# Two matrix products on TensorE in 64-row halves instead of 128 rows

## What is computed

```python
w = softmax(weight_gen, axis=-1)                  # per token and head, 7 taps
x_pad = zeros of 6 tokens, then x
out = einsum('bshk,bskhg->bshg', w, the 7 tokens up to s)
x = out.reshape(B * S, D)
h = x @ w_in                                      # 16384 x 192 by 192 x 2048
g = h * clip(h + 3.0, 0.0, 6.0) / 6.0
return g @ w_out                                  # 16384 x 2048 by 2048 x 192
```

## Time and profile before

| | us |
|---|---|
| median of 3 runs | 1226.28 |
| lowest and highest | 1226.02, 1226.76 |
| span of the profiled execution (first to last instruction) | 1224.4 |
| TensorE matmuls busy | 1194.6 (98%) |
| TensorE weight loads busy | 1083.3 (88%) |
| VectorE busy | 803.7 (66%) |
| ScalarE busy | 634.2 (52%) |
| GpSimd busy | 690.8 (56%) |

### The profile page before, as it was taken

How to read it: one execution, slowest core, us unless ns; L and a number is a source line. 1 busy time by engine, 2 the same in 40 slices (tenths; PEclk the granted TensorE clock), 3 DMA queues, 4 the chain that set the end, 5 groups by cost and what they waited for, 6 DMA issues and landing times.

```text
span 1224.4 us, 19650 instructions
## 1 busy us (share of the span) xinstructions
PE 1194.6 (98%) x6848; PEld 1083.3 (88%) x6848; DVE 803.7 (66%) x1362; ACT 634.2 (52%) x1269; POOL 690.8 (56%) x455
## 2 busy tenths in 40 slices
PE   1999999999999999999999999999999999999998
PEld 1899999999999999999999999999999999998997
DVE  7866657576665766656666575766657666566665
ACT  3455555455555555545555554555555555455554
POOL 7893854909358192762918549094581927729100
PEclk9999999999999999999999999999999999999999
DMA  6101010010101001010010100101010010100000
GB/s 179 46 22 58 20 45 13 20 58 20 58 0 65 14 20 58 0 65 13 20 58 20 45 13 20 58 20 58 0 56 22 20 58 0 65 13 13 13 14 13
DMA packets 12071, 42.08 MB, mean 34 GB/s; under 512 B 1183, under 2 KB 5279, under 8 KB 10139
## 3 DMA queue, kind: packets, MB, share of 16 engines
q1 hardware_dynamic: 12059, 41.93, 9.8%
HBM read 29.34 MB, written 12.58 MB: 34 GB/s over the span
## 4 chain that ended last, share of the span: by engine, by line
PE 96%; DVE 1%; POOL 1%; issue 0%; DMA 0%; ACT 0%; DVEq 0%; ACTq 0%
PE work L464 48%; PE sums L482 32%; PE sums L484 15%; PE work L444 2%; POOL pool_acc L154 0%; POOL pool_prod L152 0%; DVE w_in L404 0%; DMA w_raw<-weight_gen_dram 0%; DVE work L350 0%; DVE w_out L410 0%; DVE g_lo L361 0%; DVE out_stage L381 0%; POOL pool_acc L147 0%; POOL pool_prod L148 0%; DVE xt_b L373 0%
## 5 line engine op out<-in xcount | busy, mean ns | idle before, releaser
L350 DVE SCALAR_TENSOR_TENSOR work<-relu,work 128x512 f32<-128x512 f32 x512 | 355.2, 694 | 402.9 <-ACT relu L254 402.8
L482 PE MATMUL sums<-w_out,g_hi 128*128 128x384 f32 x2048 | 614.1, 356 | 0.7 <-DVE g_lo L361 0.7
L254 ACT ACTIVATE relu<-work 128x512 f32<-128x512 f32 x512 | 306.4, 598 | 554.0 <-PE work L464 549.3
L484 PE MATMUL sums<-w_out,g_lo 128*128 128x192 f32 x2048 | 513.0, 251 | 0.0
L464 PE MATMUL work<-xt_a,w_in 128*128 128x512 f32 x1536 | 449.3, 400 | 2.0 <-DVE xt_b L373 2.0
L482 PEld LDWEIGHTS sums<-w_out,g_hi 128*128 128x128 f32 x2048 | 384.3, 188 | 23.7 <-DVE g_lo L361 1.3
L484 PEld LDWEIGHTS sums<-w_out,g_lo 128*128 128x128 f32 x2048 | 389.8, 190 | 15.8
L361 DVE TENSOR_TENSOR g_lo<-work,g_hi 128x512 fp32r<-128x512 f32 x512 | 349.7, 683 | 2.1
L464 PE MATMUL work<-xt_b,w_in 128*128 128x512 f32 x1024 | 318.1, 392 | 0.0
L264 ACT CAST g_hi<-work 128x512 fp32r<-128x512 f32 x512 | 299.3, 585 | 11.4 <-DVE work L350 11.3
L147 POOL TENSOR_TENSOR pool_acc<-x_in,w_soft 128x768 f32<-128x768 f32 (+1 forms) x32 | 50.0, 1563 | 442.7 <-DVE w_soft L341 429.7
(11 more groups left out here) (31 smaller groups left out, 203.7 us busy)
## 6 DMA issues: line engine op xcount, KB each, us to landing
x_in<-x_dram SPq DMA_DIRECT2D x15, 1344.0 KB, 6.0
out_dram<-out_stage SPq DMA_DIRECT2D x32, 384.0 KB, 2.8
w_raw<-weight_gen_dram SPq DMA_DIRECT2D x16, 224.0 KB, 3.0
w_out_raw<-moe_w_out_dram SPq DMA_DIRECT2D x1, 1152.0 KB, 13.5
x_in<-x_dram SPq DMA_DIRECT2D x1, 768.0 KB, 5.1
w_in_raw<-moe_w_in_dram SPq DMA_DIRECT2D x1, 768.0 KB, 8.9
w_in_raw<-moe_w_in_dram SPq DMA_DIRECT2D x2, 384.0 KB, 10.3
w_out_raw<-moe_w_out_dram SPq DMA_DIRECT2D x1, 384.0 KB, 6.6
```

Source lines behind the costliest of these rows:

```text
L254: nc.scalar.activation(t.relu[:, m % 2, :], t.work[m % BANKS][:], ACT.Relu, bias=3.0).then_inc(s.relu_ready, 1)
L350: nc.vector.scalar_tensor_tensor(bank[:], t.relu[:, m % 2, :], 6.0, bank[:], ALU.min, ALU.mult).then_inc(s.gated, 1)
L482: nc.tensor.matmul(t.sums[n][:, 0:2 * D], t.g_hi[:, m % BANKS, cols], t.w_out[:, j, :], start=(j == 0), stop=False)
L484: ins = nc.tensor.matmul(t.sums[n][:, D:2 * D], t.g_lo[:, m % BANKS, cols], t.w_out[:, j, 0:D], start=False, stop=(j == TILES - 1))
```

## The change

TensorE works in halves of 64 rows: each matmul takes 64 of the 128 rows of both operands, the upper (0 to 63) or the lower (64 to 127). Upper and lower matmuls alternate and write different PSUM banks. Slots go in twos, a *duo* d being slots 2d and 2d + 1. For each duo TensorE does:

- `fill_first`: five rounds of (upper half of the even tile, lower half of the odd tile);
- `multiply` of two half tiles (`parts_after` lists which: part 0 and part 1 of a tile are its two halves of rows, in each of the four token blocks);
- `fill_second`: five rounds of (upper half of the odd, lower half of the even tile);
- `multiply` of the next two half tiles.

The fifth product of a fill, the low part of `w_in` for channels 128 to 191, takes only the 256 columns in which the half of rows holds the high part of x; the product of the two low parts is left out. In `multiply`, four matmuls work on two token blocks: 384 columns upper, 384 lower, 192 upper, 192 lower. A semaphore `turned` makes a `multiply` wait until the one before has ended, `filled_first` makes the second filling of a bank wait for the first. `g_hi` and `g_lo` get 6 places instead of 4. Transposes of a group are likewise in two instalments, 12 matmuls of 64 rows and 64 columns instead of 6 of 128. ScalarE and VectorE take two tiles at a time: relu, relu, high, high and gate, gate, low, low. The softmax steps hang on duos 2, 3, 4 and 5, behind slots 5, 7, 9 and 11.

The diff, cut to its core:

```diff
+G_SLOTS = 6
+DUOS = ROUND // 2
+HALF_DUOS = SLOTS // 2
+TRANSPOSE_DUO = GROUP_SLOTS.index(TA) // 2
+FIRST_DUO = 2
+SHIFT_AT, EXP_AT, SUM_AT, SCALE_AT = 2, 3, 4, 5
+ROWS = [slice(0, DB), slice(DB, P)]
...
+def parts_after(d, second_fill):
+    h = d % HALF_DUOS
+    before, recent, new = 2 * d - 4, 2 * d - 3, 2 * d - 2
+    if second_fill:
+        return {1: [(recent, 1)], 2: [(before, 1), (recent, 1), (new, 0)],
+                TRANSPOSE_DUO: [(recent, 1)], TRANSPOSE_DUO + 1: [(before, 1), (recent, 0)],
+                TRANSPOSE_DUO + 2: [(new, 0)]}.get(h, [(recent, 1), (new, 0)])
+    return {2: [(before, 0), (recent, 0)], TRANSPOSE_DUO + 1: [(before, 0)],
+            TRANSPOSE_DUO + 2: [(recent - 2, 1)]}.get(h, [(before, 1), (recent, 0)])
...
-        products = [(t.w_in[:, 0, 0, cols], t.xt_a[:, half, 0, :]), (t.w_in[:, 0, 0, cols], t.xt_a[:, half, 1, :]),
-                    (t.w_in[:, 1, 0, cols], t.xt_a[:, half, 0, :]), (t.w_in[:, 0, 1, cols], t.xt_b[:, half, :]),
-                    (t.w_in[:, 1, 1, cols], t.xt_b[:, half, :])]
-        for i, (w, x) in enumerate(products):
-            ins = nc.tensor.matmul(bank[:], w, x, start=(i == 0), stop=(i == len(products) - 1))
-        ins.then_inc(s.filled, 1)
...
+    def products(m, r):
+        half, j = slot(m)
+        bank = t.work[m % BANKS]
+        rows = ROWS[r]
+        cols = slice(j * P, (j + 1) * P)
+        hi_b = bank.rearrange("p (i o c) -> p i o c", o=2, c=P)[:, :, r, :]
+        return [(bank[:], t.w_in[rows, 0, 0, cols], t.xt_a[rows, half, 0, :]),
+                (bank[:], t.w_in[rows, 0, 0, cols], t.xt_a[rows, half, 1, :]),
+                (bank[:], t.w_in[rows, 1, 0, cols], t.xt_a[rows, half, 0, :]),
+                (bank[:], t.w_in[rows, 0, 1, cols], t.xt_b[rows, half, :]),
+                (hi_b, t.w_in[rows, 1, 1, cols], block_b(t, half, r, r))]
...
+        for i, (upper, lower) in enumerate(zip(products(2 * d, 0), products(2 * d + 1, 1))):
+            nc.tensor.matmul(*upper, start=(i == 0), stop=False)
+            ins = nc.tensor.matmul(*lower, start=(i == 0), stop=False)
+        ins.then_inc(s.filled_first, 1)
...
+        pe.wait_ge(s.filled_first, duos_filled(q, d))
+        both = list(zip(products(2 * d + 1, 0), products(2 * d, 1)))
...
+    def multiply(q, tiles, odd_first, turns, first=False, by_sets=False):
+        if turns is not None:
+            pe.wait_ge(s.turned, turns)
+        order = [(m, part, group) for m, part in tiles for group in range(2)]
...
+            sets = [(n, ROWS[(n + odd_first) % 2]) for n in (2 * group, 2 * group + 1)]
...
+                nc.tensor.matmul(t.sums[n][:, 0:2 * D], t.g_hi[rows, m % G_SLOTS, n * P:(n + 1) * P],
+                                 t.w_out[rows, j, :], start=(j == 0 and part == 0), stop=False)
+            for n, rows in sets:
+                ins = nc.tensor.matmul(t.sums[n][:, D:2 * D], t.g_lo[rows, m % G_SLOTS, n * P:(n + 1) * P],
+                                       t.w_out[rows, j, 0:D], start=False, stop=last_part)
...
+    def duo(q, d, last=False):
+        bank_free(q, 2 * d - 3, last)
+        fill_first(q, d, last)
+        starts = d % HALF_DUOS == FIRST_DUO
+        multiply(q, parts_after(d, 0), 1, None if starts else turns_before(q, d, 0), by_sets=starts)
+        fill_second(q, d, last)
+        multiply(q, parts_after(d, 1), 0, turns_before(q, d, 1))
```

## The result

The changed kernel takes 1240.18 us (median of 4 runs, 1238.66 to 1251.71) against 1226.18 for the kernel before (4 runs, 1226.02 to 1226.76). The ratio is 1.0133, 95% interval 1.0092 to 1.0174. The prediction said 1190, and had the likelier side wrong. Its range, 1080 to 1410, takes in 1240 only because it was stretched for two rivals, neither of which came; the likeliest case's own range, 1165 to 1225, doesn't. The profiled execution spans 1236.6 us, 12.2 more than the 1224.4 of before.

The account below looks back on a forecast made before the run. TensorE's own instruction stream, busy for 98% of the span, was taken as the bound. 1224.4 - 56 (fifth product) + 15 (loop's body) + 5 (longer chain) = 1188 profiled, so 1190 us for the runs; range 1080 to 1410.

Parts of the forecast that it names:

- two rivals: TensorE's halves: loads one after another, 1342 to 1537 us, chance 0.30; or hiding each other's overhead, 1034 to 1134, chance 0.12.
- the likeliest case: Whole kernel: halves run side by side with undisturbed loads; 1190 us, own range 1165 to 1225, chance 0.47.
- The loop's body: TensorE's loop: some 1820 instructions instead of 930 may need fetching at each turn; +15 us, bounds 0 and 42.
- My sign of being wrong: TensorE's second product: the prediction is wrong if it takes other than about 1.1 us a tile.
- the sign for the fetch: TensorE's loop branch: a gap right behind each turn, with instruction packets 15 times as many, would show fetching.
- Fifth product: Fill's fifth round: 256 columns wide in each half, from 0.234 to 0.117 us a tile; -56 us.
- The second product in halves: TensorE's multiply: sixteen half-row matmuls and loads a tile instead of eight, still 1.12 us if halves are independent; 0.
- Loads in line: Second product: loads of both halves wait for one another; +118 us (1342) to +312 us (1537), chance 0.30.
- Longer chain: ScalarE and VectorE taking two tiles at a time: small stalls where a group ends; +5 us, bounds 0 and 16.
- transposes: TensorE's group transposes: 24 of 64 rows a turn instead of 12 of 128, loads still 0.109 us each; 0.
- Twice as many instructions: TensorE's issue: 26 matmuls and 26 loads in 2.17 us, one instruction per 0.042 us, is permitted; cost 0.
- Gain given back to waits: Group ends stall 0.5 us each (16) and the loop's way back costs 42: 1226 us, chance 0.08.

Follow-up runs that it names:

- e5: e1 with the fifth product of each fill over all 512 columns again, low-low part included: 1237.46 us, ratio 1.0087 to the kernel before.
- e1: The changed kernel with TensorE's loop over the pairs written out as straight code: 1188.26 us, ratio 0.9687 to the kernel before.
- e3: The kernel before (128 rows) with three pairs in one turn of TensorE's loop: 1229.66 us, ratio 1.0030.
- e7: The kernel before (128 rows) with two pairs in one turn of TensorE's loop, the fifteenth pair written out: 1232.16 us, ratio 1.0045.
- e4: The kernel before (128 rows) with TensorE's loop written out: 1226.38 us, ratio 1.0006.
- e2: The changed kernel with three pairs in one turn of TensorE's loop: 1203.77 us, ratio 0.9813 to the kernel before.
- e6: e1 with each half's 384- and 192-column matmuls following one another in the second product instead of alternating halves: 1187.92 us, ratio 0.9683 to the kernel before.

## Why the prediction was wrong, point by point

The ledger by the runs: 1226.2, minus 49.2 for the fifth product (e5 to e1), plus 10.9 for all else in halves (e5 against before), plus 51.9 for the loop (the changed kernel against e1): 1239.8, where 1240.2 was measured. These are differences in one chain of runs, so that they add up proves nothing; the check that stands by itself is the 51 us read from the trace against the 51.9 of e1.

*The step that failed: "The loop's body", +15.* The mechanism was named and put in its place, and its bounds were 0 and 42. Measured is 52. Two things made it too small. The price was taken as a third of a transfer's 2.8 us, on the argument that only part of the body would be missing; the branch lasts 3.3 to 4.0 us, and the nine packets of each turn, at about 256 instructions each, are the whole body of 1800 fetched anew. And the bounds left out what follows: nine stretches at half clock, 15 us, though the trace of before has fills 0.43 us apart where TensorE begins after its idle start:

```profile
28.10 1.05 PE L464 MATMUL work<-xt_b,w_in 128*128 128x512 f32 x2
28.96 1.48 PE L464 MATMUL work<-xt_a,w_in 128*128 128x512 f32 x3
```

One thing that was left out would have made it smaller: 1.2 us of each branch are hidden under matmuls still queued. A way back that doesn't fit costs 3.7 us here. With 52 in place of 15 my own sum says 1224.4 - 56 + 52 + 5 = 1225, no change: this step took the forecast gain away. The other 13 us, from no change to slower, are the two terms below, 7 and 6 us.

My sign of being wrong stood at the wrong part. The second product came out at 1.12 us a tile (e1), as written; it was the sign for the fetch, a gap behind each turn and many more instruction packets, that came true.

*Fifth product, -56.* Right in kind, 7 us too large: 49.2. The round itself is 0.12 long against 0.22 to 0.23, as the rows at 186.52 show, so about 0.11 shorter: 58 us by the medians of e5 and e1 (0.226 and 0.113). A part doesn't arrive. In the middle of these two traces the other four rounds of a fill together take 0.01 us longer in e1 and the multiply behind it another 0.01. Why isn't shown.

*The second product in halves, 0, and "Loads in line" (0.30).* The forecast is right and the rival wrong: the halves run side by side with loads of their own. In the middle of the trace of e5 a fill takes 1.17 us and a multiply 1.11, as in the kernel before. The row I read for the load's price misled. In e1 transposes of 64 rows, each with its load, stand 0.06 apart in a half (594.30 and 594.36 below), so a load of 64 rows and 128 columns takes up at most that. Then the 0.109 between transposes of 128 rows, which also have twice the columns to stream, need not be a load's price; for loads of 128 rows no run separates the two. Between the rounds of the second product nothing changed: 0.28 from one pair of 384-column matmuls to the next.

*Longer chain, +5, and transposes, 0.* Together with start and end they came to 11 (11.7 between the profiled spans of e5 and before). In the profile of e5 the distance between two groups' transposes is 37.38 us against 37.20 before: 0.18 in each of 30 distances, 5.4 us. The first transposes behind the start come 2.9 us later (57.2 against 54.3 us), and from the last ones to the end it is 57.4 us instead of 54.0. A likely reason, not tested: at both ends two tiles at a time go through ScalarE and VectorE with little else for TensorE to do. Here is the transposes' place in e1:

```profile
594.30 0.21 PE L463 MATMUL work<-ident,attn_b 64*128 64x64 f32 x1
...
594.36 0.22 PE L463 MATMUL work<-ident,attn_b 64*128 64x64 f32 x1
594.37 0.35 PE L464 MATMUL work<-ident,attn_a 64*128 64x64 f32 x3
594.54 0.44 PE L548 MATMUL sums<-w_out,g_hi 64*128 64x384 f32 x2
594.83 0.25 PE L551 MATMUL sums<-w_out,g_lo 64*128 64x192 f32 x2
594.91 0.36 PE L548 MATMUL sums<-w_out,g_hi 64*128 64x384 f32 x2
...
596.56 0.25 PE L551 MATMUL sums<-w_out,g_lo 64*128 64x192 f32 x2
596.74 0.49 PE L512 MATMUL work<-xt_a,w_in 64*128 64x512 f32 x1
```

The instalment of transposes is over in 0.24 us, and the multiply behind it is recorded with 0.44 instead of 0.36 and takes 0.29 to its 192-column one instead of 0.20. It has the wait `turned` on the multiply before it, and here no phase of 1 us lies in between, but those 0.24. I had written that each such wait had a phase of 1 us in between; at the transposes that is wrong, at 0.1 us a time. The fill at 596.74 comes 0.18 behind the last matmul instead of 0.09, by the list of waits for low parts (4.3 us in 26 waits over the whole of e1). That the 0.18 a group is made of these is read from the rows, not shown by an experiment.

*Twice as many instructions, 0.* The issue kept up: in e1 no two matmuls start over 0.40 us apart between 41 and 1180 us. But the cover has another side, which the text didn't see: the same number of queued instructions lasts half as long, so a pause of the sequencer (which hands out the instructions) shows more: 2.5 us lost per branch in the changed kernel against 0.9 in e3 and e7, for branches of the same length.

*"Gain given back to waits" (0.08)* was the rival that came nearest: it had the way back at 42 us and 1226 as its time. Its other part, 16 us at the ends of groups, did not come: 0.18 us a group. It got too small a chance, since its price was taken as an upper bound and not as one of two values that a loop can have.

## What to carry to other kernels

Count the instructions of a loop's body before making them smaller and more. For TensorE a body of 1475 came back in 0.2 us and one of 1643 in 3.5 us, at each turn; in the bodies tried here (907 to 1811, and longer) it fitted or it didn't, so such a term has two values and no middle one. The limit lies between 1475 and 1643. If it doesn't fit, write the loop out, which cost nothing here (e4), or run more work per turn (e2: 15.5 us are left of the 51.9). Row halves are worth it where they take columns away, as the fifth product's 256 of 512 in a half, since side by side they otherwise do no better than 128 rows (e5: 11 us worse).

## What was unexpected of the hardware

- Matmuls of different row halves overtake one another: e6, with the order changed so that each waits behind the other half's, ran in 1187.92 us against 1188.26, and its timeline shows the later half's matmuls starting first.
- A taken branch to what has to be fetched lasts 3.3 to 4.0 us, with 64-row and 128-row matmuls alike. Pauses of 2.2 to 3.0 us between matmul starts were followed by 3.4 us at 1.2 GHz in nine of fourteen cases in the changed kernel and in four of four in e2. After pauses of 0.8 to 1.3 us in e3 and e7 the clock stayed at 2.4 GHz.
- The changed kernel's runs spread more (1238.66 to 1251.71) than those of before (1226.02 to 1226.76). The slowest has a mean granted clock of 0.974 against 0.985 of the profiled one; 0.011 of 1240 us is 14 us, and its span is 13.1 us longer. So more time was spent at half clock, but where isn't known, as only the profiled run's trace is kept: the five pauses that it has without a slow stretch would make 8.5 us at 1.7 each, and 13.1 are to be explained.
